# Table reads moved to the top of the round in a fused attention and two-MoE kernel

## The reference, cut to what matters

```
for e in range(E):                      # first layer; the second has another gate
    mask = expert_idx == e
    h = np.maximum(x[mask] @ w1[e], 0.0)        # 384 -> 1024
    out[mask] = gate_w[mask, None] * (h @ w2[e])   # 1024 -> 384
```

## Time and profile before

| What | Value |
|---|---|
| Median of 3 runs | 810.31 us (810.2 to 811.85) |
| Profiled execution | 813.64 us, of it 811.9 us span |
| PE busy, matmuls | 727.1 us (90%) |
| PE busy, weight loads | 638.3 us (79%) |
| DVE busy | 503.7 us (62%) |
| ACT busy | 390.8 us (48%) |
| Loop of layer 0 | 214.07 us to 502.79 us, 26 rounds |
| Loop of layer 1 | 535.13 us to 794.50 us, 27 rounds |
| Chain that ended last | PE 69%, DVE 8%, issue 8%, ACT 5% |

### The profile page before, as it was taken

The page is one execution under the profiler, slowest core; times in us unless marked ns, Lnnn a source line. Parts: engine busy times, 40 slices in busy tenths (PEclk is TensorE's granted clock), DMA queues, the critical chain, the costliest instruction groups (busy, mean ns, idle before and its releaser), DMA issues.

```text
span 811.9 us, 21320 instructions
## 1 busy us (share of the span) xinstructions
PE 727.1 (90%) x5494; PEld 638.3 (79%) x5495; DVE 503.7 (62%) x1363; ACT 390.8 (48%) x760; POOL 160.3 (20%) x202
## 2 busy tenths in 40 slices
PE   2898898980899999999999998499999999999994
PEld 2687687760688988888888887379999999999993
DVE  8899899986466674746675675544635444436621
ACT  4565777781355463535464464144534444425521
POOL 5354565553000000000000000001000000010000
PEclk9999999996799999999999999689999999999998
DMA  5655588635543351423352433233505152416110
GB/s 130 148 148 151 156 251 238 176 99 188 185 157 116 117 175 37 135 91 109 117 173 91 141 116 117 91 101 132 202 29 194 49 182 78 157 39 194 39 33 26
DMA packets 50267, 103.73 MB, mean 128 GB/s; under 512 B 7921, under 2 KB 29904, under 8 KB 50224
## 3 DMA queue, kind: packets, MB, share of 16 engines
q1 hardware_dynamic: 29536, 67.18, 26.9%
q10 hardware_dynamic: 15568, 21.76, 9.8%
q0 software_dynamic: 5120, 14.26, 4.8%
HBM read 85.73 MB, written 19.01 MB: 129 GB/s over the span
## 4 chain that ended last, share of the span: by engine, by line
PE 69%; DVE 8%; issue 8%; ACT 5%; DMA 4%; ACTq 2%; SPq 2%; POOL 1%; DVEq 0%; POOLq 0%
PE bank L1303 18%; PE bank L1329 17%; PE bank L1337 10%; PE bank L1308 9%; PE bank L1318 5%; DMA rk<-rk_in 3%; PE bank L1270 2%; PE bank L1292 2%; ACT wall L559 2%; DVE SF L765 2%; DVE Q L756 2%; PE bank L1124 1%; ACTq L246 1%; PE bank L1263 1%; POOL rkp L393 1%
## 5 line engine op out<-in xcount | busy, mean ns | idle before, releaser
L1303 PE MATMUL bank<-wall,xT_hi 128*128 (+1 forms) x660 | 180.1, 409 | 3.3 <-ACT xT_hi L651 3.3
L1329 PE MATMUL bank<-wall,hT_hi 128*128 x880 | 167.2, 341 | 0.8 <-ACT hT_hi L660 0.5
L1329 PEld LDWEIGHTS bank<-wall,hT_hi 128*128 128x128 f32 x880 | 154.6, 189 | 8.1 <-issue 5.5
L869 DVE TENSOR_TENSOR wall<-raw,wall 128x1024 f32 (+1 forms) x96 | 112.0, 1221 | 61.9 <-ACT wall L559 58.6
L1303 PEld LDWEIGHTS bank<-wall,xT_hi 128*128 128x128 f32 x660 | 119.7, 192 | 24.0 <-issue 4.0
L655 ACT ACTIVATE hs<-bank 128x512 f32<-128x512 f32 x110 | 65.1, 592 | 110.6 <-PE bank L1308 103.5
L559 ACT ACTIVATE wall<-raw 128x1024 f32 (+1 forms) x96 | 95.1, 1050 | 42.0 <-issue 42.0
L1308 PE MATMUL bank<-wall,xT_lo 128*128 (+1 forms) x330 | 94.5, 394 | 0.0
L660 ACT ACTIVATE hT_hi<-bank 128x512 fp32r<-128x512 f32 x110 | 59.8, 596 | 68.6 <-PE bank L1318 68.6
L1337 PE MATMUL bank<-wall,hT_lo 128*128 x440 | 91.0, 348 | 0.0
L1030 DVE TENSOR_TENSOR xT_lo<-bank,xT_hi 128x384 fp32r<-128x384 f32 x57 | 31.8, 558 | 87.9 <-ACT xT_hi L651 87.9
(11 more groups left out here) (194 smaller groups left out, 953.7 us busy)
## 6 DMA issues: line engine op xcount, KB each, us to landing
raw<-wall_in SPq DMA_DIRECT2D x96, 512.0 KB, 3.8
xin<-sorted ACTq DMA_DIRECT2D x59, 194.0 KB
rk<-rk_in SPq DMA_DIRECT2D x46, 192.0 KB
v_in<-v_src ACTq DMA_DIRECT2D x24, 192.0 KB
vT<-vT_in ACTq DMA_DIRECT2D x48, 96.0 KB
wb<-w_in SPq DMA_DIRECT2D x46, 96.0 KB
sorted<-padrow SPq DMA_DIRECT2D x16, 194.0 KB, 2.1
sorted<-yrow,slot POOLq DMA_INDIRECT x28, 2.6
```

Of the source, the lines that this page charges most:

```text
L869: v.tensor_tensor(w_lo[:, slot, cols], raw[:, q], w_hi[:, slot, cols].bitcast(F32), ALU.subtract).then_inc(w_split, 1)
L1303: pe.matmul(bank[n][:, :], xT_hi[:, k, :], w[:, bass.ds(slot, 1), cols].rearrange("p o n -> p (o n)"), start=(k == 0 and w is w_hi), stop= ...
L1329: pe.matmul(bank[2][:, 0:DM], hT_hi[:, j, :], w[:, bass.ds(slot, 1), W2 + j * DM:W2 + (j + 1) * DM].rearrange("p o n -> p (o n)"), start=( ...
```

## The change

PE's second pair of reads (slot and expert of tile p) moves from ahead of `second_product_hi` to the top of the round, behind the first pair and ahead of `transpose_h`. `with_next_expert` is cut in two: `next_expert` reads `e1` and `place`, both outside of the branch, and `split_next` holds the branch and what is in it. In its loop ACT calls `next_expert` for p-1 and for p at the top of the round, ahead of `copy_ht`, and the two `split_next` behind it. DVE, and ACT after its loop, call `with_next_expert` where they did; it is now the one after the other.

```diff
-        def with_next_expert(eng, m, g, split, pieces):
-
+        def next_expert(eng, m, g):
 
             e1 = eng.value_load(tab[0:1, m, bass.ds(g + TAB_FIRST + 1, 1)], min_val=0, max_val=E)
+            return e1, eng.value_load(tab[0:1, m, bass.ds(g + TAB_PLACE + 1, 1)], min_val=0, max_val=1)
+
+        def split_next(eng, m, g, following, split, pieces):
+
+            e1, place = following
             with eng.If(e1 > 0):
-                place = eng.value_load(tab[0:1, m, bass.ds(g + TAB_PLACE + 1, 1)], min_val=0, max_val=1)
                 eng.wait_ge(moes[m]["mm2"], g + 2)
                 for q in pieces:
                     split(E * m + e1, bass.ds(place, 1), q)
             with eng.Else():
                 eng.nop()
+
+        def with_next_expert(eng, m, g, split, pieces):
+            split_next(eng, m, g, next_expert(eng, m, g), split, pieces)
...
                 with act.Fori(0, last) as p:
+                    late, soon = next_expert(act, m, p - 1), next_expert(act, m, p)
                     copy_ht(p)
-                    with_next_expert(act, m, p - 1, split_hi, LATE)
-                    with_next_expert(act, m, p, split_hi, SOON)
+                    split_next(act, m, p - 1, late, split_hi, LATE)
+                    split_next(act, m, p, soon, split_hi, SOON)
...
                     slot, pieces = weights(p + 1)
+                    old_slot, old_pieces = weights(p)
                     transpose_h(p)
                     first_product(p + 1, 0, slot, pieces)
                     if m == 0:
                         transpose_y(p + 1)
-                    old_slot, old_pieces = weights(p)
                     second_product_hi(p, old_slot, old_pieces)
```

## The result

The changed kernel takes 890.77 us (median of 6 runs, 889.85 to 896.4) against 810.71 us (6 runs, 808.7 to 811.85): ratio 1.0997, 95% interval 1.097 to 1.1024. The forecast was 888 us.

What follows compares the result with a forecast made beforehand. PE's stream of weight loads was taken to bound the kernel, with reads holding sequencers. Layer 0 +42.5 us and layer 1 +33 make +77.5, so 888 us; range 850 to 908, the forecast's own 875 to 898.

Steps and rivals of the forecast that it cites:

- PE's pair at the top: Top of PE's round: four reads need 3.1 us, leaving 1.1 us of hole ahead of L1318 in layer 0, 0.3 in layer 1.
- ACT's reads: ACT ahead of copy_ht: four reads take 2.5 us, delay hT_hi; no stall at L1329 in layer 0, 0.65 us in layer 1.
- DVE's added read: DVE's two calls: reading `place` every time adds 1.45 us without splits, hidden in layer 0, 0.72 with; SOON rounds take 14.6 us.
- The sum: Whole kernel: layer 0 +42.5 us, layer 1 +33 us, together +77.5 us, for a forecast of 888 us.
- the tail: Behind layer 0's loop: two more reads on ACT while PE waits for yT, +1.2 us.
- The first (hidden reads): Rival: PE's queue hides the reads, late hT_hi and splits delay nothing, holes of 0.20 and 0.69 are won: 800 us; chance 0.05.
- The second (PE only): Rival: only PE's part counts, ACT's reads being shorter than they look or hidden: about +28, 838 us; chance 0.07.
- The third (DVE without effect): Rival: PE and ACT as summed, but DVE's splits do not reach the one-hot or `ext`: 855 us; chance 0.11.
- The clock: Rival: PE's clock falls around idle stretches in SOON rounds, 1.7 us each, eight times +14: 902 us; chance 0.12.

Runs made afterwards that it cites:

- e5: The kernel before with only DVE's read of `place` moved ahead of its branch: 819.0 us, ratio 1.0077.
- e6: The kernel before with one more read, its value unused, at the top of PE's round (three there): 826.56 us, ratio 1.0187.
- e3: The changed kernel, but DVE, and ACT behind its loop, read the slot inside the branch as before: 878.07 us, ratio 1.0796.
- e1: The kernel before with only PE's second pair of reads moved to the top of the round: 851.19 us, ratio 1.0469.
- e7: The kernel before with three more reads, values unused, at the top of PE's round (five there): 889.03 us, ratio 1.0964.
- e2: The kernel before with only ACT's four reads moved ahead of its copies of hT in its loop: 864.1 us, ratio 1.063.
- e8: The changed kernel with the slot taken as expert number modulo 2, one read a tile; against the kernel before: 806.97 us, ratio 0.9943.

## Why the prediction was right, point by point

- **PE's pair at the top.** Right. I forecast 1.1 us of hole ahead of L1318 in rounds of layer 0 behind one without splits, and 0.3 in layer 1; the trace has 1.10 and 0.35. The wait of L1275 for the one-hot, which pins PE's sequencer in layer 0, is confirmed by e5, where DVE's read alone opens a hole of 0.6 us ahead of the transposes, and by e6: the third read costs there and is free in layer 1. Rounds without splits: 11.7 us, forecast 11.75.
- **ACT's reads.** Right. In layer 0 hT_hi starts 1.71 us after the transposes (1.75) with no hole at L1329; in layer 1 the hole there is 0.78 us, not 0.65. hT_hi and L1336 are not late for this: they start 2.67 and 3.52 us after the transposes (forecast 2.7 and 3.6), and the term of about 0.2 us between them, called an estimate, is 704.08 - 703.83 = 0.25. PE is ready sooner: its loads up to L1336 take 2.74 us behind a hole, where I had the 2.90 of the kernel before. So the hole is larger and the round still shorter than forecast, 10.42 us and not 10.53.
- **DVE's added read.** Right. It is the smallest of the three (0.8% alone), and in the diff it shows only as a line that leaves the branch. SOON rounds 14.60 us (14.6), first split at 6.43 us (6.5), one-hot done at 11.0 (11.05). LATE rounds 12.3 to 12.5 us, and one of 13.2 (12.1): the term is short by 0.2 us, of which 0.15 is the first split, 4.15 us after the round's start and not 4.0. The reads that DVE makes behind its LATE splits are hidden by these, as I had it: e3, which lacks the one behind the splits, has its first split in LATE rounds at 3.9 to 4.2 us, and these rounds take 12.1 to 12.4 us at full clock. In layer 1 the hole behind a SOON round is 1.25 us longer, forecast 1.15.
- **The sum.** The loop of layer 0 +43.6 us (forecast +42.5, less 1.1), 2.2 more by the LATE rounds; the loop of layer 1 +31.8 (+32.7, the +33 without its start). Between the loops +3.2, forecast 1.2 for the tail and 0.6 for the start of layer 1. L1270's wait for yT in the tail grew from 2.19 to 3.13 us, by 0.94 and not 1.2. The rest has other places: 1.0 us where PE works behind that wait (mean granted clock 0.69, before 0.78), 0.5 us more of waiting for rows by DMA, and 0.8 us where layer 1 starts (clock 0.56, before 0.66). The start of layer 0 was forecast at +1.5 and is at -1.2; what precedes it differs by more than that between the eleven profiled executions (208.8 to 214.1 us), so nothing follows. The total of 77.4 us against 77.5 is closer than the terms are: they are off by +2.2, -0.9, +1.4 and -2.7 us, and that these cancel is luck. The medians differ by 80.1 us, so the forecast of 888 is 2.8 us low.
- **The rivals.** The first (hidden reads) would have needed PE's sequencer 1.5 us ahead; the runs show that it is never more than about 2.8 us ahead of L1318, of which two reads take 1.6. The second (PE only) is e1: 851 us, and not the 838 that I gave it, because I had left out what a later one-hot does to SOON and LATE rounds. The third (DVE without effect) is e3: 878 us, not 855, for the same reason: DVE is late there by ACT's reads already.
- **The clock.** It was the fourth rival, at 0.12, with a loss in each of the eight SOON rounds. In the loop of layer 0 it happened in one LATE round of eight, and the first SOON round began at the lower clock and was no longer for it. The argument against it was that the idle stretches here are shorter than 1.95 us; they were forecast at 1.5 and 1.7 and are 1.88 and 2.17, so that argument was wrong. In the table: us, PE, PEld, DVE, ACT, POOL busy, PEclk, DMA share, GB/s, for two LATE rounds.

```profile
482.70:495.90 13.20, 12.43 (x64) 10.76 (x65) 8.17 (x26) 6.79 (x13) 0.15 (x1) 0.87 0.41 137
444.00:456.40 12.40, 10.88 (x65) 9.70 (x65) 8.41 (x26) 6.56 (x13) 0.90 (x1) 1.00 0.47 153
```

  One of them ran at a mean granted clock of 0.87, for a part of it at 1.2 instead of 2.4 GHz, behind a SOON round with idle stretches of 1.88 and 2.17 us ahead of it, and took 0.8 us more. The seven others kept 2.4 GHz, six of them behind the same idle stretches. In e3, with 1.15 and 2.18 us, it was two of eight. So in the loops the clock is worth about 1 us here, and the idle stretch alone does not decide whether it falls; what does is open.

**How far PE's sequencer runs ahead.** It is fifteen pairs of load and matmul, some 30 instructions, in layer 1 of six kernels. With four reads at the top the loop's last instruction is 3.15 us ahead of the transposes, with five 3.8, and the holes are what this exceeds 2.8 us by: 0.35 and 0.98. Whether a full queue or something else stops the sequencer there, no run here separates.

The Trainium skill (TensorE: Matmul & The Clock Gate, section "Architectural detail: the array is 16× 32×32, not 1× 128×128") gives TensorE a queue of 64. An estimate from that figure: if all 64 could be used for instructions, they would last some 6 us where 30 last 2.8, and e7's five reads in layer 1 would be hidden. The trace does not agree: they leave a hole of 0.98 us.

## What to carry to other kernels

A read from a table into a register is 0.6 to 0.75 us of its engine's sequencer in these traces, and shows nowhere as busy time. Before moving one, find the last thing that pins that sequencer (here the semaphore of the one-hot in layer 0, the fifteen pairs handed over in layer 1) and count what of the engine's own work is still queued behind it: up to there a read is free, beyond it costs nearly its full time in every round (0.64 of 0.75 us for the fifth here). An instruction hoisted out of a branch is executed for every caller of the helper, also where the branch is not taken. Here that cost something only in rounds in which splits stood behind it; in the others, and in all of layer 1 in e5, it was hidden. And the cheapest read is the one whose value follows from another register.

## What was not expected of the hardware

The prediction had no price for each part by itself; the expectations of e1 and e2 had them right (852 and 860 us). What I would not have guessed from the busy shares: ACT, busy for 48% of the span before, costs more by four early reads (6.3%) than PE, busy for 90%, by two (4.7%). And the costs are not additive: 4.7, 6.3 and 0.8% alone make 11.8%, all together 10.0%. A register's value modulo 2 cost nothing that can be seen: in e8, where PE's sequencer is pinned by the one-hot, two reads and two modulos put the transposes 286.25 - 284.17 = 2.08 us behind its end, the 0.5 + 1.6 us of two reads alone. (Rounds of 9.58 us in layer 1 would not show it, since a third read is free there too.)
